# Weight segments in dead buffers: a ring of eleven, seven matrices loaded in attention, eight first layers and then eight second ones

## The reference

```
attention: q, k, v (4 batches, 8 heads, 768 positions, 64), chunks of 32 queries,
           each sees 16 positions left of its chunk, 8 right of it, and 8 memory rows
x = its output as (3072 tokens, 512)
soft MoE:  logits = x @ phi                        # 32 slots, 4 for each of 8 experts
           d = softmax over tokens; slot_input = d.T @ x
           for e: h = max(slot_input[e] @ w1[e], 0); slot_out[e] = h @ w2[e]
           c = softmax over slots; x = c @ slot_out
top-1 MoE: e = argmax(x @ w_gate); gate = softmax weight * sigmoid(x @ w_output_gate)[e]
           out = gate * (max(x @ w1[e], 0) @ w2[e])
```

## Time and profile before

| | |
|---|---|
| median of the runs | 565.82 us |
| profiled execution | 566.25 us, of which span 564.5 us |
| TensorE busy | 501.7 us (89%) |
| VectorE, ScalarE, GpSimd busy | 214.7, 201.6, 135.0 us |
| chain by engine | TensorE 72%, DMA 12%, ScalarE 5%, VectorE 4%, issue 3% |
| largest chain parts | L760 39%, weight transfers 11% |
| DMA | 97.89 MB, mean 173 GB/s |
| attention, to its last V product | 0 to 192 us |
| slot stage, to slot_out_t | 203.5 to 257.5 us |
| routing, to the first tile's second layer | 257.5 to 302.9 us |
| tiles | 302.9 to 558 us |

### The profile page before, as it was taken

One profiled execution on the slowest core, in us unless ns is written; L12 is line 12 of the kernel. 1 busy time (PEld: TensorE's weight loads), 2 busy tenths in 40 slices (PEclk: granted clock), 3 DMA queues, 4 the chain that ended last, 5 costly groups with the idle time before them and its releaser, 6 DMA issues.

```text
span 564.5 us, 11392 instructions
## 1 busy us (share of the span) xinstructions
PE 501.7 (89%) x3728; PEld 298.6 (53%) x3729; DVE 214.7 (38%) x974; ACT 201.6 (36%) x769; POOL 135.0 (24%) x128
## 2 busy tenths in 40 slices
PE   3799999999998788766857999999999999999993
PEld 3688777777776533235553444444444444444441
DVE  3677777777776360004912221222212222122210
ACT  1798898888887311111000111111111111111110
POOL 2243343332433100000520221222122221222210
PEclk9999999999998969896756999999999999999998
DMA  9998999999965299999994634781011100110000
GB/s 138 173 188 237 182 262 245 197 262 223 216 204 169 94 370 311 335 378 403 398 397 179 236 123 169 220 295 38 33 39 39 39 29 30 40 40 2 3 0 0
DMA packets 122416, 97.89 MB, mean 173 GB/s; under 512 B 95680, under 2 KB 96176, under 8 KB 122384
## 3 DMA queue, kind: packets, MB, share of 16 engines
q1 hardware_dynamic: 115600, 77.70, 50.7%
q10 hardware_dynamic: 3168, 12.58, 6.3%
q0 software_dynamic: 3616, 7.20, 3.9%
HBM read 90.78 MB, written 8.52 MB: 176 GB/s over the span
## 4 chain that ended last, share of the span: by engine, by line
PE 72%; DMA 12%; ACT 5%; DVE 4%; issue 3%; POOL 1%; ACTq 1%; SPq 0%; POOLq 0%; DVEq 0%
PE bank L760 39%; DMA arena<-in_moe_w_dram 11%; PE bank L584 5%; PE bank L554 5%; PE bank L517 4%; PE bank L744 4%; PE bank L560 3%; ACT arena L1044 3%; PE bank L532 2%; PE bank L726 2%; PE bank L713 2%; PE bank L542 1%; DVE arena L832 1%; ACT shared L1050 1%; DMA arena<-rows_scratch,tok_sorted 1%
## 5 line engine op out<-in xcount | busy, mean ns | idle before, releaser
L760 PE MATMUL bank<-arena 128*128 x496 | 225.9, 603 | 0.0
L760 PEld LDWEIGHTS bank<-arena 128*128 128x128 f32 x496 | 90.2, 191 | 103.6 <-issue 100.1
L452 POOL TENSOR_TENSOR arena<-arena,row_inv 96x1024 f32<-96x1024 f32 x32 | 60.6, 1893 | 120.6 <-DVE row_inv L825 120.6
L485 POOL DMA_INDIRECT out_dram<-arena,tok_sorted x31 | 31.4, 1013 | 195.3 <-ACT arena L1141 195.3
L1011 DVE TENSOR_SCALAR arena<-bank 128x256 f32<-128x256 f32 x124 | 43.9, 416 | 63.9 <-PE bank L744 63.9
L1141 ACT ACTIVATE arena<-bank,gate_sorted 128x512 f32<-128x512 f32 x31 | 21.3, 687 | 103.6 <-PE bank L760 103.6
L832 DVE CUSTOM_DVE_ANT_0 arena<-bank,masks 96x128 f32<-96x128 f32 x256 | 55.0, 277 | 4.3 <-PE bank L517 4.3
L1134 ACT COPY arena<-bank 128x128 f32<-128x128 f32 x31 | 8.2, 265 | 119.2 <-PE bank L735 119.2
L1044 ACT ACTIVATE arena<-arena,neg_max 96x128 f32<-96x128 f32 x128 | 49.8, 393 | 1.7 <-issue 1.5
L1053 ACT ACTIVATE arena<-arena,neg_max 96x128 f32<-96x128 f32 x128 | 49.8, 395 | 0.0
L1019 DVE COPY arena<-arena 128x128 f32<-128x128 f32 x31 | 7.8, 252 | 95.2 <-DMA arena<-rows_scratch,tok_sorted 95.2
(11 more groups left out here) (161 smaller groups left out, 560.7 us busy)
## 6 DMA issues: line engine op xcount, KB each, us to landing
arena<-in_moe_w_dram SPq DMA_DIRECT2D x26, 2048.0 KB, 10.4
arena<-in_moe_w_dram ACTq DMA_DIRECT2D x6, 2048.0 KB, 10.5
arena<-in_k_dram SPq DMA_DIRECT2D x32, 240.0 KB
arena<-in_v_dram SPq DMA_DIRECT2D x32, 240.0 KB
arena<-in_q_dram SPq DMA_DIRECT2D x32, 192.0 KB
arena<-in_mem_k_dram SPq DMA_DIRECT2D x32, 16.0 KB
arena<-in_mem_v_dram SPq DMA_DIRECT2D x32, 16.0 KB
arena<-rows_scratch,tok_sorted POOLq DMA_INDIRECT x31, 3.5
```

Of the source, the lines that this page charges most:

```text
L452: g.tensor_tensor(probs[:, t % 4], probs[:, t % 4], row_inv[:, t % 2, :].unsqueeze(2).to_broadcast([TQ, H, NK]), ALU.mult).then_inc(p_norm ...
L485: pool.indirect_dma_start(out=out, out_offset=bass.IndirectOffsetOnAxis(ap=tok_sorted[:, j:j + 1].bitcast(U32), axis=0), in_=o_sb[:, j % 2 ...
L760: ins = mm(bank[4 + par][:, :], h_t[:, par, f * 128:(f + 1) * 128], w2_all[:, bass.ds(e * SEG + f * DM, DM)], start=(f == 0), stop=(f == K ...
```

## The change

The ring gets eleven segments, PRE becomes 7. The seventh matrix (up 6) is issued by ScalarE after step 32, outside its loop. `units` is all eight ups, then all eight downs. To make room, k_t and q_t move from `shared` into the segment of V, the probabilities and V change segments, `shared` shrinks, and the routing's buffers and hot_tok move into segment 10, which holds the tiles' buffers in the tail. The relu multiplies by a column of `own_slots` (1 where the row's slot belongs to the expert, else 0), so that rows of other experts' slots are zero, and one PSUM bank can sum the second layers of all experts. ScalarE copies it once, and one fold of 32 columns makes all slots.

```diff
-    RING = 10
+    RING = 11
     KQV = 4
     LAG = 8
-    PRE = 6
+    PRE = 7
...
-    units = [("up", e) for e in range(PRE)]
-    for pr in range(E // 2):
-        if PRE + 2 * pr < E:
-            units += [("down", 2 * pr), ("down", 2 * pr + 1), ("up", PRE + 2 * pr), ("up", PRE + 2 * pr + 1)]
-        else:
-            units += [("down", 2 * pr), ("down", 2 * pr + 1)]
-    SLOT_UNITS = len(units)
+    units = [("up", e) for e in range(E)] + [("down", e) for e in range(E)]
     place = {u: i % RING for i, u in enumerate(units)}
 
 
     for e in range(E):
-        place[("hidden", e)] = 4 + (e + 2) % 4
+        place[("hidden", e)] = (5, 6, 7, 8, 9)[e % 5]
...
-        v_in = work[:, SEG:SEG + 4 * DM].rearrange("p (r c) -> p r c", r=KQV)
-        probs = work[0:TQ, 2 * SEG:3 * SEG].rearrange("p (r h c) -> p r h c", r=4, h=H)
+        v_in = work[:, 2 * SEG:2 * SEG + 4 * DM].rearrange("p (r c) -> p r c", r=KQV)
+        turned = work[:, 2 * SEG + 4 * DM:3 * SEG]
+        k_t = turned[:, 0:H * NK].rearrange("p (r c t) -> p r c t", r=2, c=H // 2)
+        q_t = turned[:, H * NK:H * NK + H * TQ].rearrange("p (r c t) -> p r c t", r=2, c=H // 2)
+        probs = work[0:TQ, SEG:2 * SEG].rearrange("p (r h c) -> p r h c", r=4, h=H)
...
         hid_t = part(2 * 512, "p (r c) -> p r c", r=2)
-        combine_t = shared[:, taken[0]:taken[0] + NT // 4 * TQ].rearrange("p (g t) -> p g t", g=NT // 4)
-        g_all = part(E * GF, "p (e f) -> p e f", e=E)
-        r_le = part(NR * E, "p (j e) -> p j e", j=NR)[0:1]
+        out_parts = part(512, "p (a c) -> p a c", a=1)
+        hid_rows_b = part(512, "p (a c) -> p a c", a=1)
+        combine_t = shared[:, 0:NT // 4 * TQ].rearrange("p (g t) -> p g t", g=NT // 4)
+        slot_out_4 = shared[:, NT // 4 * TQ:NT // 4 * TQ + KD * 4 * NS].rearrange("p (c r s) -> p c r s", c=KD, r=4)
+        g_all = shared.rearrange("p (e f) -> p e f", e=E)
...
+        hid_rows = [hid_rows_a[:, 0, :], hid_rows_b[:, 0, :]]
+        own_slots = sb("own_slots", [128, E // 2])
...
-        tail = arena[:, 8 * SEG:10 * SEG]
+        tail = arena[:, 10 * SEG:11 * SEG]
...
+                    sp.wait_ge(p_turned, NT)
+                elif i == PRE + 2:
                     sp.wait_ge(weighted, NT)
-                elif i == PRE + 2:
-                    sp.wait_ge(p_turned, NT)
...
             def down(e):
                 arrived(("down", e))
                 pe.wait_ge(hid_copied, e // 2 + 1)
-                if e >= 2:
-                    pe.wait_ge(down_copied, e - 1)
                 w = matrix(("down", e))[1]
                 for half in range(2):
                     for m in range(4):
                         at = m * 128 + (2 * (e % 2) + half) * NS
-                        ins = mm(bank[6 + e % 2][32 * m:32 * m + NS, :], hid_t[:, e // 2 % 2, at:at + NS],
-                                 w[:, 4 * half + m, :], start=(half == 0), stop=(half == 1))
+                        ins = mm(bank[6][32 * m:32 * m + NS, :], hid_t[:, e // 2 % 2, at:at + NS],
+                                 w[:, 4 * half + m, :], start=(e == 0 and half == 0), stop=(e == E - 1 and half == 1))
                 ins.then_inc(down_made, 1)
 
-            def pick(e):
-                pe.wait_ge(down_copied, e + 1)
-                for c in range(KD):
-                    ins = mm(bank[2][:, c * NS + e * SPE:c * NS + (e + 1) * SPE], out_parts[:, e % 2, c * 128:(c + 1) * 128],
-                             fold[:, e * SPE:(e + 1) * SPE], start=True, stop=True)
-                ins.then_inc(folded, 1)
-
             up(0)
-            for pr in range(E // 2):
-                if pr + 1 < E // 2:
-                    up(pr + 1)
-                turn_hidden(pr)
-                for e in (2 * pr, 2 * pr + 1):
-                    down(e)
-                    if e >= 1:
-                        pick(e - 1)
-            pick(E - 1)
+            up(1)
+            turn_hidden(0)
+            up(2)
+            turn_hidden(1)
+            up(3)
+            down(0)
+            down(1)
+            turn_hidden(2)
+            down(2)
+            down(3)
+            turn_hidden(3)
+            for e in range(4, E):
+                down(e)
+            pe.wait_ge(down_copied, 1)
+            for c in range(KD):
+                ins = mm(bank[2][:, c * NS:(c + 1) * NS], out_parts[:, 0, c * 128:(c + 1) * 128], fold[:, :], start=True, stop=True)
+            ins.then_inc(folded, 1)
...
+            for half in range(2):
+                link(vec.tensor_reduce(own_slots[64 * half:64 * half + 64, :],
+                                       fold[64 * half:64 * half + 64, :].rearrange("p (r a b) -> p r a b", a=2, b=SPE)[:, :, half, :],
+                                       AX.X, ALU.add))
...
-                vec.tensor_scalar(hid_rows[:, pr % 2, :], bank[3 + pr % 2][:, :], 0.0, None, ALU.max).then_inc(relu_made, 1)
-            dve.wait_ge(folded, E)
+                vec.tensor_scalar(hid_rows[pr % 2], bank[3 + pr % 2][:, :], 0.0, own_slots[:, pr:pr + 1],
+                                  ALU.max, ALU.mult).then_inc(relu_made, 1)
+            dve.wait_ge(folded, 1)
...
+                e = EARLY * (B - 1) + j - LAG - TPB * (B - 1)
+                if e < PRE:
+                    dst, src = matrix(("up", e))[::-1]
+                    act.dma_start(dst, src).then_inc(early_in, 16)
...
-                for e in (2 * pr, 2 * pr + 1):
-                    act.wait_ge(down_made, e + 1)
-                    if e >= 2:
-                        act.wait_ge(folded, e - 1)
-                    sc.copy(out_parts[:, e % 2, :], bank[6 + e % 2][:, :]).then_inc(down_copied, 1)
+            act.wait_ge(down_made, E)
+            sc.copy(out_parts[:, 0, :], bank[6][:, :]).then_inc(down_copied, 1)
```

62 lines of the change are left out of this document (30 added, 32 removed).

## The result

| | before | after |
|---|---|---|
| median of 4 runs, us | 565.24 (564.61 to 566.05) | 556.33 (555.46 to 557.99) |
| profiled execution, span, us | 566.25, 564.5 | 557.99, 556.2 |

The ratio of the times is 0.984, with an interval of 0.981 to 0.987: 8.9 us faster, where 5.6 were forecast (560.2 us). The time lies inside the stated range (555.5 to 563.5), nearer to rival A's 556.7 than to the forecast. A second measurement of both kernels gave 0.986, 7.7 us. (Ahead of the prediction stood 565.82 for the kernel before, a median of three.)

The account below looks back on a forecast made before the run. The slot stage was taken as bound by weight bytes, ending when the last down matrix lands. -5.86 us there and +0.3 for the fold gave -5.6 us, so a median of 560.2 us, range 555.5 to 563.5.

Parts of the forecast that it names:

- rival A: Slot stage: down matrices slow through TensorE's traffic, not their kind; five at 5.07 us each, time 556.7 us; chance 0.17.
- Step 2: Slot stage: five matrices instead of six left behind the first pair's product; last down matrix lands 5.86 us earlier.
- L: Moment when the last down matrix has landed, end of the slot stage's transfers: 251.88 us before, 246.0 forecast.
- Step 1: Attention: seventh early matrix (up 6) issued by ScalarE; its bytes are hidden, its issue costs +0.41 us.
- Step 3: Slot stage: all first layers, then all second; no gain of its own, since transfers end last.
- Step 4: Behind the last down product: one copy and one fold of 32 columns take 2.2 us, +0.3 us.
- Rival B: TensorE's clock slower from 233 us to the last landing; gain 2.3 to 3.5 us, time 562.5 us; chance 0.15.
- Rivals C and D: C: no change, later stage takes gain back, 565.8 us, chance 0.05; D: q_t, k_t in arena slow attention, 569.8 us, 0.06.
- step 6: Attention: buffers moved, q_t and k_t into the arena; nothing, either sign at most 2.6 us over 32 steps.

Follow-up runs that it names:

- r_before: The kernel before, unchanged, measured again for a second trace; ratio to the kernel before 0.998 [0.995, 1.002].
- e_rows4k: Changed kernel, with down loads filled from the up matrices in rows of 4 KB, not 2 KB (only times count); ratio to the kernel before 0.976.
- e_up6_late: Changed kernel, but up 6 is loaded behind attention by the sync queue, not early by ScalarE; ratio to the kernel before 0.980.
- e_before_onesum: Kernel before with only the one sum added (mask in relu, one PSUM bank, one copy, one fold); ratio to the kernel before 1.001.
- e_down0_late: Changed kernel, but down 0 waits for the last V product again, as down 1 does; ratio to the kernel before 0.988.
- e_ahead3: Changed kernel with three transfers in flight in place of two; ratio to the kernel before 0.986.
- e_picks: Changed kernel without the one sum: copy and fold behind each down product, one copy buffer; ratio to the kernel before 0.985.
- v_ahead3: Changed kernel with up 6 behind attention, down matrices in 8 KB runs and three transfers in flight; ratio to the kernel before 0.979.

## Why the prediction was nearly right, step by step

**Step 2, the release.** Right in mechanism and, for the first traces, in size: -5.77 - 0.5 = -6.27 from slot_in_t to S0, against 48.74 - 42.49 = -6.25. The second pair of traces gives -10.8, of which a good part is r_before's slow end; so that the two numbers agree to 0.02 is luck, since traces of one kernel differ by more. L was put at 246.0; the matrix landed at 243.46, and the 2.5 between are attention (-2.15 where +0.41 was forecast). The sync queue's three loads behind attention show the steps before that. The kernel after (start us, us, engine, line, operation):

```profile
189.79 0.38 SPq L408 DMA_DIRECT2D arena<-in_moe_w_dram  x1
197.51 0.38 SPq L408 DMA_DIRECT2D arena<-in_moe_w_dram  x1
207.29 1.49 SPq L408 DMA_DIRECT2D arena<-in_moe_w_dram  x2
```

These are down 1, down 2 and, at the release, down 3 and 4; down 0 had gone at 186.9 (189.5 forecast). I said that the queue would be "nearly dry" at the release; two of the three matrices ahead had landed by 202.98, and the third landed at 208.34 (210.5 forecast). The first pair behind it had landed 18.5 us after the release, within my limit of 20. The pace I took, 5.77 us a down matrix, held for this kernel: 11.63 and 11.47 for two.

**What the pace is made of.** I weighed only two causes, the kind of matrix and TensorE's traffic. In the last link e_rows4k decides for the kind, at 5.1 against 5.77. But rows of 2 KB went at 5.4 there in other kernels of the same bytes (e_up6_late, e_before_onesum and e_down0_late, 10.70 to 10.81 for two) and at up to 7.0 (r_before), and rows of 4 KB are not always at 5.1: in e_before_onesum two of the hidden matrices landed 6.1 us apart. So of the 0.7 us above 5.1 some 0.3 belongs to the rows by my estimate (5.4 less 5.1), and the rest changes from one execution to the next. That e_up6_late and e_ahead3, which keep more in flight, are at 5.4 fits a better filled queue, and isn't shown to be that. The Trainium skill, "DMA: Bandwidth & Descriptors", section "Specifications", sets 512 B as the size from which the rate is full; rows of 2 KB and 4 KB both pass, and in the last link here they differ, 5.35 us or more a matrix against 5.09: the measurement decides against it.

**Step 1, the seventh early matrix.** Its bytes were hidden, as I said, but nothing came of it: I took them out of the queue behind attention, and e_up6_late shows that they were not missing there. The matrix that stopped counting behind the release is the one for which the eleventh segment was free. The cost was also off: +0.41 forecast. ScalarE's load lies beside a copy that ran anyway; the kernel after:

```profile
177.04 0.48 ACT L1074 COPY x_t<-bank 128x384 f32<-128x384 f32 x1 [0.73 <-PE bank L585]
177.05 0.41 ACTq L1106 DMA_DIRECT2D arena<-in_moe_w_dram  x1
177.56 0.40 ACT L1049 ACTIVATE arena<-arena,neg_max 96x128 f32<-96x128 f32 x1
```

Of the table's attention times the short ones divide into 141.85 to 141.91 with the load and 141.67 to 141.76 without it, 0.15 us; the long ones are 143.27 to 143.38 with it and 143.27 and 143.31 without. The -2.15 seen in the first traces is not the change's: 1.42 of it is the clock at 180 to 184 us, which four of the other traces, one of them of the kernel after itself, share with the first trace of before, and 0.74 is the moment of ScalarE's first load, which lies anywhere between 47.0 and 49.7 us in the traces.

**Step 3, the order.** Right that it has no gain of its own as long as transfers end last. That they do rests on the one sum, which I didn't say: in e_picks, with copies and folds in single file, TensorE's chain is 2.7 us longer than the transfers.

**Step 4, one sum.** +0.3 forecast. By S0 to slot_out_t it is -0.1 and -2.1 in the two pairs, by time nothing (1.001). Behind the last product I took 2.2 us and 1.78 passed, 0.59 for the copy and 1.09 for the fold: my lower bound.

**Rival B, the clock.** It came, and it was too small to matter. Granted over 232 to 236 was 0.65; the last three downs took 2.48, 3.64 and 3.56 us. The kernel after, TensorE in order of time:

```profile
231.97 2.48 PE L658 MATMUL bank<-arena,shared 128*32 128x512 f32 x16 [2.97 <-DMA arena<-in_moe_w_dram]
...
237.63 3.64 PE L658 MATMUL bank<-arena,shared 128*32 128x512 f32 x16 [3.18 <-DMA arena<-in_moe_w_dram]
...
243.51 3.56 PE L658 MATMUL bank<-arena,shared 128*32 128x512 f32 x16 [2.23 <-DMA arena<-in_moe_w_dram]
```

Where the clock was full in the last down (v_ahead3: 1.92 us), slot_out_t follows S0 by 3.7 us in place of 5.4, so half clock costs 1.7 us there. But the kernel before paid the same 3.62, so no difference came from it. Where the fold fell at half clock too, as B had it (e_up6_late: 1.92), slot_out_t was 6.30 us behind S0, 0.9 more than in the kernel after: B's price was right for the fold, and its gain of 2.3 to 3.5 was not, since the release brought its whole size. The Trainium skill, "TensorE: Matmul & The Clock Gate", section "HAM oscillation", has the clock drop between bursts that wait for transfers: the trace of the kernel after agrees for this place, at 0.65, but in v_ahead3 the last down ran at full clock behind a wait of 1.5 us.

**Rivals C and D, step 6.** False. The stages behind slot_out_t stand at 45.9 and 252.1 (45.4 and 252.3). Products that read the moved buffers take no longer; the kernel after has 289 ns where the earlier trace rows has 293:

```profile
L518 PE MATMUL bank<-arena 64*96 64x128 f32 x512 | 37.6, 289 | 4.8 <-DVE arena L860 4.8
```

**What the forecast missed,** by the first traces' spans (8.34 us gained, 5.56 forecast): -2.56 in attention, 0.3 of it a mis-sized cost and the rest the clock and the start, -0.44 in the fold, and +0.2 behind slot_out_t. The medians are 8.9 and 7.7 apart; their intervals begin at 7.3 and 5.7 us, so a gain beyond the forecast's 5.6 is likely real. Where it lies isn't shown: the stage from slot_in_t to S0 gained 6.0 to 7.4 us, by the 48.53 and 48.74 of e_before_onesum and the first trace of before and the 42.49 and 41.35 of the kernel after. The terms that were mis-sized are step 1's cost, +0.41 where 0 to 0.15 was measured, and step 4's +0.3, where the first traces have -0.1. That the time came near rival A's 556.7 is luck: the pace that A asked for, 5.07 us a down matrix, did not come.

## To carry to other kernels

Where a stage is bound by transfers that wait for a buffer, count the transfers that stand behind the release, and keep the queue filled until it comes; a transfer made earlier still only makes the queue run dry sooner. Look at the length of a contiguous run before the number of bytes: here the last two matrices of 2 MB took 5.35 us or more each in rows of 2 KB, 5.09 in rows of 4 KB and 4.94 in runs of 8 KB. And take a second trace of both kernels before a difference of 1 to 2 us in a stage is explained: here attention alone moved by 1.6 us with the place at which the clock fell, in both kernels.

## What was unexpected of the hardware

- With two or three in flight and clear of other writes, 2 MB took 5.4 to 7.0 us of the queue in rows of 2 KB, 5.1 to 5.7 in rows of 4 KB (e_rows4k) and 4.9 to 5.9 in runs of 8 KB, by the lengths of transfer links; only at the end of the stage were the longer runs faster in every trace.
- The write of 384 KB beside the weights cost the stage 3 to 4 us; with the write moved, the first gather came 5.8 us behind its indices, not 0.8, and the time was the same. Neither size is explained by its bytes.
- The clock falls at other places in other executions of the same kernel: over 244 to 248 us it was 1.00 in the first trace of before, and over 246 to 250 it was 0.50 in the second, at the same place of the work. The five traces with such a fall at 180 to 184 us have an attention 1.4 to 1.7 us longer than the nine without.
